# Second MLP on one core: the turn of a tile's rows moved behind the turn of the features of the tile two places ahead of it

## The chip, the cores and the metric

One core of one Trainium2 chip. The metric is the device time of one execution in microseconds (us), as the median of several runs.

## The reference

```python
def _attn_ref(r, k, v, w, u):            # (4, 8, 768, 48)
    for t in range(S):
        cur = einsum('bhd,bhe->bhde', u[None] * kt, vt)
        y[:, :, t] = einsum('bhd,bhde->bhe', rt, state + cur)
        state = wt[:, :, :, None] * state + einsum('bhd,bhe->bhde', kt, vt)

def _moe_ref(x, w_in, w_out):            # 3072 tokens, 384 -> 2048 -> 384
    h = x @ w_in
    return maximum(0.01 * h, h) @ w_out

def _moe2_ref(x, expert_emb, tau, w1, w2):   # 8 experts, 384 -> 1024 -> 384
    logits = (xn @ en.T) / tau               # xn, en: rows of unit length
    expert_idx = argmax(logits, axis=1)
    gate_w = softmax(logits)[expert_idx]
    for e in range(8):
        mask = expert_idx == e
        out[mask] = gate_w[mask, None] * (maximum(x[mask] @ w1[e], 0) @ w2[e])
```

A linear attention with decays feeds a dense MLP, and its output feeds a second MLP in which each token goes through one of eight experts. The change lies in the second MLP.

## The kernel before

Each engine has its own instruction stream, and the streams meet in semaphores. The attention and the first MLP are interleaved until about 557 us; then comes the second MLP. Its tokens are sorted by expert into tiles of 128 rows. In the profiled execution 28 tiles (0 to 27) are used. The first K1 = 5 are rows of an expert that is picked early, while the first MLP still runs. Tiles 5 to 23 stand in a loop with two tiles per turn (`tiles`, with tile 5 ahead of the loop), and tiles from NT = 24 on in nested branches (`last_tiles`), since their number depends on the data. MT = 34 is the most that there can be.

All products run as three fp32r matmuls (high x high, high x low, low x high) in place of one fp32 matmul, so every operand is split into a high and a low half: ScalarE copies the high half, VectorE subtracts it to get the low one.

One tile j goes like this:

- POOL gathers its 128 rows of 384 numbers by an indirect DMA into `xg`, which has two places (`gather`, L766, for tiles 0 to 4; `fetch`, L781, from tile 5 on). The list of rows comes into `idr` by a DMA of SP (`load_ids`, L516). A gather waits until the tile two places before has been turned (`s_xgT`).
- TensorE turns the rows with three transposes into one PSUM bank, X_BANK = 7 (`turn_g`, L1049). It waits for the gather (`s_xg`) and until the previous tile's rows have left the bank (`s_xgh`, `s_xgl`).
- ScalarE copies them to `xgh` (`x_hi2`, L1391), and VectorE makes `xgl` (`x_lo2`, L1831).
- `features(j)`: two halves of 9 matmuls of 512 columns (`feature_half`, L1067), out into the A banks. It waits for `xgh`, `xgl` and the expert's weights. ScalarE takes them out with a relu into `hs` (L1397).
- `turn_h(j)`: eight transposes (L1084) of `hs` into the H banks; ScalarE and VectorE split them into `hh` and `hl` (L1401, L1838).
- `result(j)`: 24 matmuls of 384 columns (L1103). ScalarE scales them by the gate (`scaled`, L1409) and POOL scatters them to the output (L789).

TensorE works one tile deep. Its `tile(j)` is features(j) with the turn of the rows of tile j+1 at its end, then result(j-1), then turn_h(j). ScalarE's and VectorE's `tile(j)` have x_hi2(j+1) and x_lo2(j+1) in a fixed place: behind the two relus on ScalarE, and behind the first two pieces of weights on VectorE.

Where tile j+1 has another expert than the tile two places before, SP loads its weights in four pieces into `stage` (L526), ScalarE copies the high halves (L1374) and VectorE makes the low ones (L1816): pieces 0 and 1 (for the features) at the start of tile j, pieces 2 and 3 at its end. SP loads a piece once both engines are through with the piece before it.

`start_moe` writes out tiles 0 and 1 by hand, with the last group's routing between them.

Of the kernel before, what the change touches and what calls it, by code (L numbers as in the profile page):

```python
# [23 lines left out]
def build(nc, r, k, v, w, u, w_in, w_out, emb, tau, w1, w2, out):  # L24
# [7 lines left out]
    TOK = B * S  # L32
    NT = TOK // P
    E, _, F2 = w1.shape
    FT2 = F2 // P
    GT = 3
# [4 lines left out]
    MT = K1 + (TOK - EARLY_GROUPS * GN // E + E * (P - 1)) // P  # L41
# [13 lines left out]
    with ctx:  # L55
# [299 lines left out]
        def whole(j):  # L355

            return isinstance(j, int)
# [64 lines left out]
        def routes(first, G):  # L422

            return G if first == 0 else EARLY_GROUPS - 1 + G
# [452 lines left out]
        def _(pe):  # L877
# [141 lines left out]
            def rank(r, bk, col):  # L1019

                pe.wait_ge(s_oh, r + 1)
                pe.matmul(bank[bk][:, col:col + GT * E], tri[:], r8[3][:].rearrange("p n e -> p (n e)"), start=True, stop=True)
                pe.matmul(bank[bk][:, col + GT * E:col + 2 * GT * E], ones[:], r8[3][:].rearrange("p n e -> p (n e)"),
                          start=True, stop=True).then_inc(s_rm, 1)

            def turn_x2(g, banks_):

                for i in range(GT):
                    pe.wait_ge(s_oe, GT * g + i + 1)
                    for k_ in range(KT):  # L1030
                        mm = pe.transpose(bank[banks_[i]][:, k_ * P:(k_ + 1) * P], x2s[:, i, k_ * P:(k_ + 1) * P], ident[:])
                    mm.then_inc(s_x2t, 1)

            def logit_sums(z, bk):

                pe.wait_ge(s_embt, 16 * KT)
                pe.wait_ge(s_x2e, GT * (z + 1))
                for i in range(GT):
                    for k_ in range(KT):
                        mm = pe.matmul(bank[bk][:, F_LOGIT + i * E:F_LOGIT + (i + 1) * E], x2T[:, i, k_ * P:(k_ + 1) * P],  # L1040
                                       embT[:, k_, :], start=(k_ == 0), stop=(k_ == KT - 1), skip_group_check=True)
                mm.then_inc(s_lgm, 1)

            def turn_g(j, s_, half):
                pe.wait_ge(s_xg[s_], 16 * (half + 1))
                pe.wait_ge(s_xgh, j)
                pe.wait_ge(s_xgl, j)
                for k_ in range(KT):
                    mm = pe.transpose(bank[X_BANK][:, k_ * P:(k_ + 1) * P], xg[:, s_, k_ * P:(k_ + 1) * P], ident[:])  # L1049
                mm.then_inc(s_xgT, 1)  # L1050

            def feature_half(j, s_, a):

                early_ = whole(j) and j < K1
                (w1h, w1l), _ = views(eh, el) if early_ else expert(s_)
                pe.wait_ge(s_xgh, j + 1)
                pe.wait_ge(s_xgl, j + 1)
                if early_:
                    pe.wait_ge(s_phi, a + 1)
                    pe.wait_ge(s_plo, a + 1)  # L1060
                else:
                    pe.wait_ge(s_ehi, 4 * (j - K1) + a + 1)
                    pe.wait_ge(s_elo, 4 * (j - K1) + a + 1)
                pe.wait_ge(s_hs, 2 * j)
                for k_ in range(KT):
                    for n_, (x_, w_) in enumerate(((xgh, w1h), (xgh, w1l), (xgl, w1h))):
                        mm = pe.matmul(bank[A_BANK[a]][:], x_[:, k_, :], w_[:, a, k_, :],  # L1067
                                       start=(k_ == 0 and n_ == 0), stop=(k_ == KT - 1 and n_ == 2))
                mm.then_inc(s_h2, 1)

            def features(j, s_, half):

                feature_half(j, s_, 0)
                feature_half(j, s_, 1)
                if not whole(j) or j + 1 < MT:
                    turn_g(j + 1, 1 - s_, half + s_)

            def turn_h(j):
                for a in range(2):
                    pe.wait_ge(s_hs, 2 * j + a + 1)  # L1080
                    pe.wait_ge(s_hhi, 2 * j)
                    pe.wait_ge(s_hlo, 2 * j)
                    for f in range(4):
                        mm = pe.transpose(bank[H_BANK[a]][:, f * P:(f + 1) * P], hs[:, a, f * P:(f + 1) * P], ident[:])  # L1084
                    mm.then_inc(s_hT, 1)

            def result(j, s_):
                early_ = whole(j) and j < K1
                _, (w2h, w2l) = views(eh, el) if early_ else expert(s_)
                if not whole(j) or j > 1:  # L1090
                    pe.wait_ge(s_o2e, j - 1)
                for a in range(2):
                    pe.wait_ge(s_hhi, 2 * j + a + 1)
                    pe.wait_ge(s_hlo, 2 * j + a + 1)
                    if early_:
                        pe.wait_ge(s_phi, a + 3)
                        pe.wait_ge(s_plo, a + 3)
                    else:
                        pe.wait_ge(s_ehi, 4 * (j - K1) + a + 3)
                        pe.wait_ge(s_elo, 4 * (j - K1) + a + 3)  # L1100
                    for f in range(4 * a, 4 * a + 4):
                        for n_, (h_, w_) in enumerate(((hh, w2h), (hh, w2l), (hl, w2h))):
                            mm = pe.matmul(bank[R_BANK[s_]][:, 0:DM], h_[:, f, :], w_[:, f, :],  # L1103
                                           start=(f == 0 and n_ == 0), stop=(f == FT2 - 1 and n_ == 2))
                mm.then_inc(s_o2, 1)

            def tile(j, s_, half):

                features(j, s_, half)
                result(j - 1, 1 - s_)  # L1110
                turn_h(j)

            def mlp(first, lo, hi):
                for n in range(lo, hi):
                    G, f = place(first, n)
                    if G < NG:
                        if first and f == 0:
                            turn_x(G)
                        feature(first, n)
                    if not first:  # L1120
                        for m in at(sum_at, n):
                            sums(m)
                        for m in at(turn_w_at, n):
                            turn_w(m)
                        for m in at(turn_at, n):
                            turn_rk(m)
                        for m in at(score_at, n):
                            scores(m)
                    if f == 2 and 2 <= G < NG:
                        pe.wait_ge(s_g0, n)  # L1130
                        rank(routes(first, G) - 2, *route_bank(first, G, n))
                    if G == NG - 1:
                        if f == 2:
                            turn_x2(n // FT - 1, TURN6)
                        if f == 4:
                            logit_sums(0, LOGIT6)
                        if f == 7:
                            rank(routes(first, G) - 1, *route_bank(first, G, n))
                        if f == 12:
                            turn_g(0, 0, 0)  # L1140
                    if n >= lo + LAG or (not first and n >= LAG):
                        out_part(n - LAG)
                    if not first and n == SECOND - 2:
                        pe.wait_ge(s_vs, 1)
                        pe.wait_ge(s_yhi, NC)
                        pe.wait_ge(s_ylo, NC)
                        pe.matmul(bank[STEADY[2]][:, 0:1], ones[:], violsum[:], start=True, stop=True
                                  ).then_inc(s_vt, 1)

            def start_moe(first, hi):  # L1150

                feature_half(0, 0, 0)
                turn_x2((hi - LAG) // FT - 1, TURN7)
                feature_half(0, 0, 1)
                turn_g(1, 1, 0)
                logit_sums(1, LOGIT7)
                turn_h(0)
                features(1, 1, 0)
                rank(routes(first, NG - 1), RANK7, F_LOGIT + GT * E)
                result(0, 0)  # L1160
                turn_h(1)
                for j in range(2, K1):
                    tile(j, j % 2, j // 2)

# [38 lines left out]
            def all_tiles():  # L1203

                n_used = used_tiles(pe)
                tiles(pe, tile)
                last_tiles(pe, n_used, lambda j: tile(j, j % 2, j // 2), lambda n: result(n - 1, (n - 1) % 2))
# [833 lines left out]
```

## Time and profile before

| | us |
|---|---|
| median of 3 runs | 840.05 (839.87 to 840.52) |
| the profiled execution | 839.8 |
| its span, first to last instruction | 838.0 |
| TensorE busy in the span | 820.6 |

The profiled execution's time is its span and 1.8 us around it. Times in the rows count from the start of the span. PE is TensorE's matmuls, PEld its weight loads, DVE is VectorE, ACT is ScalarE, POOL is GpSimd, SP is SyncE. Matmuls are pipelined: the time from one start to the next is what one costs, and it is less than the duration shown.

### The profile page before, as it was taken

The page shows a single profiled execution, that of the slowest core. Times are in us where ns is not written, and L with a number is a line of the kernel's source. Part 1 is how long each engine was busy: PE and PEld are TensorE (multiplying, and loading weights), DVE is VectorE, ACT ScalarE, POOL GpSimd, SP SyncE. Part 2 cuts the span into 40 slices and gives each one's busy share as a digit, 9 for nine tenths or more (in the row PEclk, how much of TensorE's full clock was granted, in tenths as well). Part 3 has the DMA queues.
Part 4 walks back from the last instruction along what each step waited for, and adds up shares of the span by engine and source line. Part 5 has one row for each costly group of instructions (what it writes and reads, how often), then busy time and mean ns, then how long its engine had stood idle before and what let it go on. Part 6 is the DMA issues. An engine that isn't in the chain of part 4 may idle for free.

```text
span 838.0 us, 17878 instructions
## 1 busy us (share of the span) xinstructions
PE 820.6 (98%) x5709; PEld 770.7 (92%) x5709; DVE 547.8 (65%) x1296; ACT 439.9 (52%) x924; POOL 203.8 (24%) x286
## 2 busy tenths in 40 slices
PE   6999999999999999999999999999999999999996
PEld 5899999999999999999999999999989998898896
DVE  6888687678789688779778755636462512545463
ACT  5675464364464475465446435554563533565573
POOL 5511111121103012112112001312363323334423
PEclk9999999999999999999999999999999999999999
DMA  9991121264231221132110001514531512475382
GB/s 206 233 240 37 39 70 35 52 101 61 54 67 39 41 70 38 39 70 51 38 25 31 1 15 31 169 38 121 181 124 38 185 47 94 138 257 202 109 295 62
DMA packets 141289, 78.52 MB, mean 94 GB/s; under 512 B 111470, under 2 KB 129237, under 8 KB 141074
## 3 DMA queue, kind: packets, MB, share of 16 engines
q1 hardware_dynamic: 132386, 64.79, 30.2%
q0 software_dynamic: 4544, 10.85, 4.0%
q10 hardware_dynamic: 4272, 1.82, 1.0%
q8 instruction: 43, 0.70, 0.4%
q14 instruction: 44, 0.36, 0.2%
HBM read 112.90 MB, written 11.63 MB: 149 GB/s over the span
## 4 chain that ended last, share of the span: by engine, by line
PE 91%; ACT 2%; issue 2%; SPq 2%; DVE 1%; DMA 1%; POOL 0%; DVEq 0%; ACTq 0%; POOLq 0%
PE bank L1015 24%; PE bank L994 23%; PE bank L1067 13%; PE bank L1103 13%; PE bank L887 3%; PE bank L920 3%; PE bank L948 3%; PE bank L1084 3%; PE bank L943 2%; PE bank L928 1%; PE bank L1049 1%; PE bank L957 1%; SPq L439 1%; DMA stage<-in_moe_w_dram 1%; DMA wraw<-in_moe_w_in_dram 1%
## 5 line engine op out<-in xcount | busy, mean ns | idle before, releaser
L994 PE MATMUL bank<-xhl,WRh 128*128 128x384 f32 x768 | 218.3, 338 | 0.2 <-issue 0.2
L1360 ACT COPY gw<-bank 128x384 f32<-128x384 f32 x128 | 61.6, 481 | 158.7 <-PE bank L994 158.4
L994 PEld LDWEIGHTS bank<-xhl,WRh 128*128 128x128 f32 x768 | 141.2, 188 | 0.4 <-issue 0.4
L1015 PE MATMUL bank<-WRh,gh 128*128 128x384 f32 x384 | 136.4, 355 | 0.0
L994 PE MATMUL bank<-xhl,WRl 128*128 128x384 f32 x384 | 130.1, 339 | 0.0
L1015 PE MATMUL bank<-WRh,gl 128*128 128x384 f32 x384 | 129.7, 338 | 0.0
L1015 PE MATMUL bank<-WRl,gh 128*128 128x384 f32 x384 | 129.6, 337 | 0.0
L1663 DVE SCALAR_TENSOR_TENSOR gw<-gw 128x384 f32<-128x384 f32 x128 | 72.9, 570 | 62.1 <-ACT gw L1360 62.1
L1670 DVE TENSOR_TENSOR gl<-gw,gh 128x384 fp32r<-128x384 f32 x128 | 78.9, 616 | 47.2 <-ACT gh L1366 44.9
L1366 ACT CAST gh<-gw 128x384 fp32r<-128x384 f32 x128 | 65.4, 511 | 70.5 <-DVE gw L1663 58.2
L1838 DVE TENSOR_TENSOR hl<-bank,hh 128x512 fp32r<-128x512 f32 x56 | 36.1, 686 | 84.8 <-ACT hh L1401 84.5
L714 POOL TENSOR_TENSOR St<-Sx,FL 128x256 f32<-128x256 f32 x20 | 12.3, 614 | 292.4 <-DVE Sx L1644 229.7
L1683 DVE CUSTOM_DVE_ANT_0 junk<-x2s,embb 128x384 bf16<-128x384 f32 x144 | 76.5, 574 | 0.0
L1015 PEld LDWEIGHTS bank<-WRh,gh 128*128 128x128 f32 x384 | 72.3, 188 | 1.4 <-issue 0.7
L1015 PEld LDWEIGHTS bank<-WRl,gh 128*128 128x128 f32 x384 | 72.4, 189 | 0.0
L1816 DVE TENSOR_TENSOR WRl<-stage,WRh 128x1536 fp32r<-128x1536 f32 x36 | 61.8, 1756 | 15.9 <-ACT WRh L1374 15.9
L994 PEld LDWEIGHTS bank<-xhl,WRl 128*128 128x128 f32 x384 | 72.2, 188 | 0.0
L1015 PEld LDWEIGHTS bank<-WRh,gl 128*128 128x128 f32 x384 | 72.1, 188 | 0.0
L1103 PE MATMUL bank<-WRh,hh 128*128 128x384 f32 x184 | 63.9, 347 | 1.1 <-DVEq L1827 1.1
L1409 ACT ACTIVATE os<-bank,gcol 128x384 f32<-128x384 f32 x28 | 16.3, 583 | 88.1 <-PE bank L1103 88.1
L1103 PE MATMUL bank<-WRl,hh 128*128 128x384 f32 x184 | 62.0, 337 | 0.0
L1103 PE MATMUL bank<-WRh,hl 128*128 128x384 f32 x184 | 61.9, 336 | 0.0
(196 smaller groups left out, 1635.5 us busy)
## 6 DMA issues: line engine op xcount, KB each, us to landing
stage<-in_moe_w_dram SPq DMA_DIRECT2D x96, 768.0 KB
Wn<-in_w_dram SPq DMA_DIRECT2D x24, 192.0 KB, 2.7
Kn<-in_k_dram SPq DMA_DIRECT2D x24, 192.0 KB, 3.5
Vn<-in_v_dram SPq DMA_DIRECT2D x24, 192.0 KB, 3.1
x_moe<-x2s SPq DMA_DIRECT2D x24, 192.0 KB, 2.7
Rn<-in_r_dram SPq DMA_DIRECT2D x21, 192.0 KB, 3.4
wraw<-in_moe_w_out_dram SPq DMA_DIRECT2D x4, 768.0 KB, 7.3
eraw<-in_moe_w_dram SPq DMA_DIRECT2D x4, 768.0 KB, 8.8
```

Source lines behind the costliest of these rows:

```text
L887: mm = pe.transpose(bank[bk][:, h * P:(h + 1) * P], src[:, m % NSLOT, 2 * h:2 * h + 2, :].rearrange("p h d -> p (h d)"), ident[:])
L994: mm = pe.matmul(bank[F_BANK[n % 2]][:, 0:GN], win(t_)[:, f // 4, k_, cols], xhl[G % 2][:, a, k_, :], start=(k_ == 0 and n_ == 0), stop=(k ...
L1015: mm = pe.matmul(bank[O_BANK[i]][:, 0:DM], a[:, z, cols], wout(t_)[:, f, :], start=(f == 0 and n_ == 0), stop=(f == FT - 1 and n_ == 2))
L1067: mm = pe.matmul(bank[A_BANK[a]][:], x_[:, k_, :], w_[:, a, k_, :], start=(k_ == 0 and n_ == 0), stop=(k_ == KT - 1 and n_ == 2))
L1103: mm = pe.matmul(bank[R_BANK[s_]][:, 0:DM], h_[:, f, :], w_[:, f, :], start=(f == 0 and n_ == 0), stop=(f == FT2 - 1 and n_ == 2))
L1360: act.copy(gw[:, n % 2, :], bank[F_BANK[n % 2]][:, 0:GN]).then_inc(s_g0, 1)
L1366: act.copy(gh[:, n % GS, :], gw[:, n % 2, :]).then_inc(s_ghi, 1)
L1663: dve.scalar_tensor_tensor(gw[:, z, :], gw[:, z, :], 0.01, gw[:, z, :], ALU.mult, ALU.max).then_inc(s_g1, 1)
L1670: dve.tensor_tensor(gl[:, n % GS, :], gw[:, n % 2, :], gh[:, n % GS, :].bitcast(F32), ALU.subtract).then_inc(s_glo, 1)
L1683: dve.tensor_tensor_reduce(junk[:, m % 2, :], x2s[:, i, :], embb[:, e, :], 1.0, 0.0, ALU.mult, ALU.add, logits[:, GT * G + i, e:e + 1]).th ...
L1816: dve.tensor_tensor(sel(w1l, w2l), src, sel(w1h, w2h).bitcast(F32), ALU.subtract).then_inc(s_elo, 1)
L1838: dve.tensor_tensor(lo, bank[H_BANK[a]][:], hi.bitcast(F32), ALU.subtract).then_inc(s_hlo, 1)
```

## The change

In TensorE's stream alone, the turn of rows leaves its place between `features` and `result`. It now stands behind `turn_h(j)` and turns the rows of tile j+2. For tiles from NT on, where it is not known whether there is a next tile, it stands in front of the features and turns tile j+1, which is the same place in the sequence. In `start_moe` the turn of rows 2 stays where it was, and that of rows 3 moves up behind turn_h(1).

```diff
@@ features @@
                 feature_half(j, s_, 0)
                 feature_half(j, s_, 1)
-                if not whole(j) or j + 1 < MT:
-                    turn_g(j + 1, 1 - s_, half + s_)
@@ tile @@
+                maybe_last = whole(j) and j >= NT
+                if maybe_last and NT < j < MT - 1:
+                    turn_g(j + 1, 1 - s_, half + s_)
                 features(j, s_, half)
                 result(j - 1, 1 - s_)
                 turn_h(j)
+                if not maybe_last:
+                    turn_g(j + 2, s_, half + 1)
@@ start_moe @@
                 features(1, 1, 0)
+                turn_g(2, 0, 1)
                 rank(routes(first, NG - 1), RANK7, F_LOGIT + GT * E)
                 result(0, 0)
                 turn_h(1)
+                turn_g(3, 1, 1)
```

## Rows read from the trace of the kernel before

**Rows 1.** The page: busy time of an engine, and TensorE's granted clock in 40 slices.
```profile
PE 820.6 (98%) x5709; PEld 770.7 (92%) x5709; DVE 547.8 (65%) x1296; ACT 439.9 (52%) x924; POOL 203.8 (24%) x286
...
PEclk9999999999999999999999999999999999999999
```
**Rows 2.** Busy us (and instructions) of each engine by stretch, granted clock, DMA share, GB/s.
```profile
594.59:604.09 9.50, 9.50 (x57) 8.67 (x55) 5.18 (x5) 5.86 (x9) 3.41 (x6) 1.00 0.45 146
...
748.35:758.53 10.18, 9.84 (x56) 8.70 (x55) 8.52 (x7) 8.99 (x13) 5.73 (x5) 1.00 0.79 268
...
562.50:565.60 3.10, 3.10 (x30) 3.06 (x29) 0.77 (x3) 2.60 (x5) 1.05 (x1) 1.00 0.00 0
```
**Rows 3.** Waits from 590 us on: waiter, releaser, us in total, times, longest.
```profile
PEld bank L1067 <- issue: 2.5, 4, 0.9
...
PEld bank L1103 <- issue: 1.4, 1, 1.4
```
**Rows 4.** Timeline of a steady tile on TensorE: start, us, line, operation, count.
```profile
704.47 0.40 PE L1067 MATMUL bank<-WRh,xgl 128*128 128x512 f32 x1
704.71 0.49 PE L1049 MATMUL bank<-ident,xg 128*128 128x128 f32 x3
704.95 0.42 PE L1103 MATMUL bank<-WRh,hh 128*128 128x384 f32 x1
705.21 0.34 PE L1103 MATMUL bank<-WRl,hh 128*128 128x384 f32 x1
...
709.22 1.03 PE L1084 MATMUL bank<-ident,hs 128*128 128x128 f32 x8
710.01 0.48 PE L1067 MATMUL bank<-WRh,xgh 128*128 128x512 f32 x1
710.33 0.40 PE L1067 MATMUL bank<-WRl,xgh 128*128 128x512 f32 x1
```
**Rows 5.** Timeline of POOL: the gathers of tiles 4, 5, 6 and 18.
```profile
578.48 1.20 POOL L766 DMA_INDIRECT xg<-x_moe,idall  x1 [0.16 <-issue]
...
592.24 1.07 POOL L781 DMA_INDIRECT xg<-x_moe,gi  x1 [0.92 <-POOL gi L777]
...
597.93 1.85 POOL L781 DMA_INDIRECT xg<-x_moe,gi  x1 [0.92 <-POOL gi L777]
...
706.07 1.06 POOL L781 DMA_INDIRECT xg<-x_moe,gi  x1 [0.91 <-PE bank L1049]
```
**Rows 6.** Gathers, issue to landing: tile 4's, 5's, 6's, and all 26 of L781.
```profile
DMA to landing us min/median/max: 7.8/7.8/7.8
...
DMA to landing us min/median/max: 3.2/3.2/3.2
...
DMA to landing us min/median/max: 6.2/6.2/6.2
...
DMA to landing us min/median/max: 3.0/3.2/8.1
```
**Rows 7.** Timeline of SP's queue: the first four pieces of expert weights.
```profile
578.04 3.28 SPq L526 DMA_DIRECT2D stage<-in_moe_w_dram  x4
```
**Rows 8.** Timeline of TensorE: the ends of tiles 2, 3 and 4.
```profile
584.30 1.03 PE L1084 MATMUL bank<-ident,hs 128*128 128x128 f32 x8
...
593.80 1.03 PE L1084 MATMUL bank<-ident,hs 128*128 128x128 f32 x8
...
603.30 1.03 PE L1084 MATMUL bank<-ident,hs 128*128 128x128 f32 x8
```
**Rows 9.** Timeline around the wait in front of tile 21's features.
```profile
754.19 3.42 DVE L1816 TENSOR_TENSOR WRl<-stage,WRh 128x1536 fp32r<-128x1536 f32 x2
...
757.15 1.03 PE L1084 MATMUL bank<-ident,hs 128*128 128x128 f32 x8
...
757.53 0.55 DVE L1831 TENSOR_TENSOR xgl<-bank,xgh 128x384 fp32r<-128x384 f32 x1
...
758.53 0.49 PE L1067 MATMUL bank<-WRh,xgh 128*128 128x512 f32 x1 [0.35 <-issue]
```

## The prediction

> **What bounds the kernel now.** I read the page first: TensorE is busy for 98% of the span at the full granted clock [rows 1]. Then the busy time by stretch of the second MLP: an ordinary tile lasts 9.50 us and TensorE is busy in all of it, a tile with late expert weights lasts 10.18 us with 9.84 us busy [rows 2]. Then the list of waits from 590 us to the end: TensorE's weight loads stand still in front of the features (L1067) 4 times, 2.5 us together, and once more, 1.4 us, in front of the last result [rows 3]. So TensorE's own instructions set the end. Whatever the change gives or takes on them counts in full, and a new wait on TensorE counts in full too, unless a later one of those five takes it back.
>
> **What the change moves.** No instruction is added or removed: tiles 0 to 28 have their rows turned before and after, three transposes each. Before, tile j runs features(j), turn of rows j+1, result(j-1), turn_h(j). After, it runs features(j), result(j-1), turn_h(j), turn of rows j+2. So eleven transposes stand together, and each turn of rows comes earlier by one result and one turn_h. Two things follow. What a block of transposes costs beyond its transposes is paid once a tile instead of twice. And the gathered rows must have landed 5.1 us earlier than now: a result (24 x 0.174 = 4.2) and a turn_h (0.9), both from [rows 4].
>
> **The saving per tile.** The steady tile [rows 4] shows starts. The block of three begins at 704.71, the result at 704.95; the first result matmul takes 0.26 us to the second, where the other 23 take (709.22 - 705.21) / 23 = 0.174. Cost of the block: 0.24 + 0.26 - 0.17 = 0.33 us, 0.11 per transpose. The block of eight: 709.22 to 710.01 is 0.79, the first feature matmul takes 0.32 instead of about 0.235, together 0.875 us, 0.109 per transpose. The longer first matmul behind a block (0.09) is thus paid for by the last transpose, which takes only some 0.03 to the next start (0.79 - 7 x 0.109): a switch costs next to nothing. Eleven transposes cost 11 x 0.109 = 1.20 against 0.33 + 0.875 = 1.21 us. I take 0.01 us a tile; about 20 of the tiles lie where it isn't swallowed by a wait: **-0.2 us**. The bounds are 0 and, if each block of three really cost its 0.09, 26 x 0.09 = 2.3 us.
>
> The block of eleven lasts 1.2 us. A stretch of 3.1 us that was nothing but transposes and 8-column matmuls ran at clock 1.00, the upper of the two levels, and so did the tiles around it [rows 2], so I take nothing for the clock. The Trainium skill (TensorE: Matmul & The Clock Gate, Part 4: PE-mode transpose) says that transposes do not count as busy for the clock. If eleven in a row dropped it to 1.2 GHz and cost only their own doubling, that would be 26 x 1.2 = 31 us; the trace speaks against it, and it is a rival below.
>
> **Are the rows there in time?** In the steady part, yes: the gather issued at 706.07 is tile 18's [rows 5], and its new turn comes behind turn_h(16), one tile of 9.6 us after turn_h(15) at 709.22 [rows 4], so at 719.7. Gathers land 3.2 us after issue in the median and 8.1 at most [rows 6], so by 714.2. At the start it is tighter, since the first gathers stand behind the routing. Tile 4's gather is issued at 578.48 [rows 5] and lands 7.8 us later [rows 6], at 586.28. It stands beside the first four pieces of expert weights, 768 KB each, which SP issues from 578.04 on [rows 7]; later gathers land in 3.2. Before, its turn came behind features(3), 18 x 0.235 = 4.2 us into tile 3. After, it comes right behind turn_h(2), which starts at 584.30 and is over at 584.30 + 0.875 = 585.17 [rows 8]. TensorE waits 586.28 - 585.17 = 1.1 us, and some 0.1 until the first transpose goes. Behind that wait in TensorE's queue stand the five waits of features(3), which no longer run ahead; the three transposes (0.33 us) cover most of them, I take 0.1. **+1.3 us.** Its bounds: 0 if the gather came in 3.2 us, and 2.2 if it came 0.5 us later and nothing of the waits were covered (0.4).
>
> By the Trainium skill (DMA: Bandwidth & Descriptors, Queues, rings and completion order) each DMA engine takes turns between its queues, packet by packet, so a gather on POOL's queue should not stand behind SP's weights. By this rule it would land in about 3 us; the 7.8 us of [rows 6] go against it. This is a rival too.
>
> Tile 5's gather is issued at 592.24 and lands 3.2 us later, at 595.44 [rows 5, 6]. It waits for its row list, not for TensorE, so it does not move. Its turn is wanted behind turn_h(3): 593.80 + 0.88 = 594.67 [rows 8], plus the delay of 1.3, 595.97. No further wait, but without the first it would cost 0.8. Tile 6's gather follows result(2), so it moves with TensorE: 597.93 + 6.2 = 604.13 against turn_h(4)'s end at 603.30 + 0.88 = 604.18, both plus 1.3. That is even to 0.05 us; a little of it would be taken back by the wait in front of features(6). Later ones have room.
>
> **The four waits in front of the features.** They are in front of tiles 6, 21, 23 and 27 by the timeline. In the one at 758.5, tile 21's [rows 9], VectorE works through its splits of expert weights and only then makes xgl (757.53 + 0.55 = 758.08); the features start 0.45 us later, which is TensorE's sequencer with the waits that stood behind. That chain starts from turn_h two tiles before. Since the rows' turn in the middle of the tile is gone, turn_h comes 0.33 us earlier relative to the features, so the chain ends 0.33 us earlier. But the turn of rows j+2 waits for the same xgl (one bank, X_BANK) and now stands between it and the features: +0.33 if nothing overlaps, +0.2 if its transposes run under the 0.45 us of sequencer time, +0.5 where the loop's entry comes in between too (tile 6). Three of the four chains are independent (tiles 6, 21, 27; tile 23's starts from the same turn_h as tile 21's ends). I take +0.2, -0.1 and +0.1: **+0.15 us** in all, bounds -1.0 and +0.6. The wait in front of the last result is untouched: turn_h(27), ScalarE's copy, VectorE's subtraction follow each other as before.
>
> **Bookkeeping of the moved turn.** Features(2) starts 0.33 us late, as rows 3 are turned ahead of it, and the last tile gives that back, since no turn stands behind features(27). Nothing in all. ScalarE's copy of the rows (x_hi2) stands behind both relus as before and finds its input ready. POOL's gather waits for the turn two tiles before; it can only start earlier.
>
> **Sum.** -0.2 + 1.3 + 0.15 = +1.25 us on the profiled execution's 839.8, 841.05. The median of the runs is 0.25 above that execution, so 841.3.
>
> **The rivals.**
> 1. *Forecast*: one new wait of about 1.2 us ahead of features(3), the rest even. 841.3, own range 840.6 to 842.0. Chance 0.60.
> 2. *The chains' 0.33 us stay saved*: the transposes hide under the sequencer's 0.45 us. 840.05 + 1.3 - 0.2 - 1.0 = 840.15. For it: the 0.45 us is there in three of the waits. Against: the features' own waits are still behind the transposes in the queue. 0.13.
> 3. *Tile 4's gather is early, tile 5's waits instead*: 0.8 + 0.15 - 0.2, 840.8. 0.07.
> 4. *More gathers late*: tile 6's lands 7.8 us after issue like tile 4's, 1.6 us later than now; 1.5 wait, 0.5 taken back in front of features(6): 842.3. It decides from any landing above 6.3 us. 0.13.
> 5. *Other side, faster*: a switch costs TensorE its 0.09 us on the way in and on the way out, 26 x 0.18 = 4.7 us saved, less 1.45: 836.8. It gets under 838.4 from 0.12 us a tile on. Against: blocks of three and of eight cost the same per transpose. 0.06.
> 6. *The clock falls in the block of eleven*: +31 us, 871. 0.01.
>
> **Numbers.** A measurement of this kernel can tell about 0.2%, 1.7 us, from no change: 838.4 to 841.7. Faster: rival 5, 0.06. Slower: rivals 4 and 6 and about a fifth of the first, 0.27. Within: 0.67. Range 839.4 to 842.7: it takes in cases 1 to 4 with their bounds and leaves out 5, 6 and the far ends.
>
> **What would show it.** In the new profile TensorE stands still some 1.2 us ahead of its transposes L1049 near 585.2, where it now has none; the transposes stand as 8 + 3, with one longer matmul behind them; a steady tile is 0.01 us shorter; the waits in front of tiles 6, 21, 23 and 27 end with xgl, then three transposes, then the features. The forecast is wrong if tile 4's rows land before 585.2, if a steady tile changes by over 0.05 us (26 times 0.05 is 1.3), or if waits appear ahead of L1049 in the steady part, which would mean that the gathers have less room than I worked out.

## The result

The changed kernel takes 841.82 us (median of 12 runs, 840.89 to 843.75) against 840.29 us of the kernel before, run beside it; the ratio is 1.002, with a 95% interval of 1.0012 to 1.0027. That is 1.5 us slower by the medians (1.0 to 2.3 by the interval), at the edge of what can be told from no change. The forecast was 841.3, 1.25 us over its base. A second measurement (e10 below) gave 1.0017 (1.0008 to 1.0026).

In the profile after, the page's chain that ended last has one entry that the kernel before does not have, the gather that fetches rows by `idall`:

```profile
PE bank L1015 24%; PE bank L994 22%; PE bank L1067 13%; PE bank L1101 13%; PE bank L887 3%; PE bank L920 3%; PE bank L948 3%; PE bank L1082 2%; PE bank L943 2%; PE bank L928 1%; PE bank L1049 1%; PE bank L957 1%; DMA xg<-x_moe,idall 1%; SPq L439 1%; DMA wraw<-in_moe_w_in_dram 1%
```

(turn_h is now L1082 and the result L1101.) TensorE's timeline at the end of tile 2, to hold against [rows 8]: the eight transposes start at 584.66, the rows' three only at 586.98, with the gather named as what was waited for.

```profile
584.66 1.03 PE L1082 MATMUL bank<-ident,hs 128*128 128x128 f32 x8
586.98 0.55 PE L1049 MATMUL bank<-ident,xg 128*128 128x128 f32 x3 [1.29 <-DMA xg<-x_moe,idall]
587.28 0.47 PE L1067 MATMUL bank<-eh,xgh 128*128 128x512 f32 x1
```

Without a wait L1049 would have started 0.87 us behind 584.66, at 585.53: the wait is 1.45 us. POOL issued that gather at 578.83, and it landed 8.1 us later (7.8 in [rows 6]); SP's weights had started 0.46 us ahead of it:

```profile
578.83 1.19 POOL L766 DMA_INDIRECT xg<-x_moe,idall  x1 [0.16 <-issue]
```
```profile
DMA to landing us min/median/max: 8.1/8.1/8.1
```
```profile
578.37 1.60 SPq L526 DMA_DIRECT2D stage<-in_moe_w_dram  x3
```

At the end of tile 4 there is a small wait for tile 6's rows (0.2 us) and a larger one behind it, which the forecast does not have: three transposes at 606.26, the features only at 607.14, 0.88 us later where 0.25 is usual.

```profile
605.20 1.03 PE L1082 MATMUL bank<-ident,hs 128*128 128x128 f32 x8
606.26 0.55 PE L1049 MATMUL bank<-ident,xg 128*128 128x128 f32 x3
607.14 0.48 PE L1067 MATMUL bank<-WRh,xgh 128*128 128x512 f32 x1 [0.33 <-issue]
```

The view of line 368 shows why. TensorE's sequencer (PEldq) reads the number of used tiles there once, between tiles 4 and 5. In the kernel after it does so at 606.3, when the turn in front has just been released; in the kernel before at 601.6, under the result's matmuls. The first two rows are of after, the last one of before.

```profile
L368 PEldq TENSOR_LOAD <-used x1: 310/310/310, 606.3 to 606.3; - x1
...
L368 PEldq FUSED_REGOPS  x1: 156/156/156, 606.6 to 606.6; - x1
```
```profile
L368 PEldq TENSOR_LOAD <-used x1: 314/314/314, 601.6 to 601.6; - x1
```

A steady tile, to hold against [rows 4]. The result now starts without a longer first matmul (0.17 to the second), and the block is 8 + 3 transposes with one longer matmul behind it (712.46 to 712.78):

```profile
707.18 0.34 PE L1101 MATMUL bank<-WRh,hh 128*128 128x384 f32 x1
707.35 0.34 PE L1101 MATMUL bank<-WRl,hh 128*128 128x384 f32 x1
...
711.34 1.04 PE L1082 MATMUL bank<-ident,hs 128*128 128x128 f32 x8
712.22 0.49 PE L1049 MATMUL bank<-ident,xg 128*128 128x128 f32 x3
712.46 0.48 PE L1067 MATMUL bank<-WRh,xgh 128*128 128x512 f32 x1
712.78 0.40 PE L1067 MATMUL bank<-WRl,xgh 128*128 128x512 f32 x1
```

The wait in front of tile 21, to hold against [rows 9]: xgl ends at 759.63 + 0.55 = 760.18, then the three transposes, then the features 0.57 us behind xgl, where it was 0.45.

```profile
759.23 1.03 PE L1082 MATMUL bank<-ident,hs 128*128 128x128 f32 x8
...
759.63 0.55 DVE L1836 TENSOR_TENSOR xgl<-bank,xgh 128x384 fp32r<-128x384 f32 x1
...
760.32 0.52 PE L1049 MATMUL bank<-ident,xg 128*128 128x128 f32 x3
...
760.75 0.50 PE L1067 MATMUL bank<-WRh,xgh 128*128 128x512 f32 x1
```

The following table comes from the timelines. It counts each tile's first feature matmul from that of tile 0 (557.41 in before, 557.75 in after) and subtracts the same count in the first profile of the kernel before. Columns t3 to t27 are those tiles, "result" is the first matmul of the last result, and the last column is the mean length of tiles 8 to 19 in us. Rows e1 to e12 are the experiments below.

```
us later than before   t3     t4     t5     t6     t20    t21    t27   result  steady tile
after                 +1.86  +1.87  +2.71  +2.21  +2.07  +1.88  +1.41  +1.20   9.577
before (absolute)     27.68  37.18  46.68  56.74 190.95 201.12 260.16 271.11   9.587
e1  late start         0.00   0.00   0.00  +0.49  +0.36  +0.18  -0.28  -0.58   9.577
e2  only start        +1.50  +1.71  +2.10  +1.39  +1.38  +2.02  +1.48  +1.48   9.587
e3  gather 4 early    +0.35  +1.48  +1.46  +1.46  +1.34  +1.14  +0.78  +0.47   9.577
e4  lists first       +0.35  +0.37  +1.21  +0.70  +0.54  +0.35  -0.18  -0.51   9.577
e5  three blocks      +0.04  +0.09  +0.12  +0.12  -0.14  -0.13  -0.50  -0.51   9.567
e6  used early        +1.41  +1.77  +1.76  +1.76  +1.63  +1.44  +1.43  +1.13   9.577
e7  lists + used      +0.35  +1.59  +1.59  +1.63  +1.50  +1.30  +0.89  +0.59   9.577
e8  before again       0.00   0.00   0.00   0.00   0.00  +0.01  -0.43  -0.41   9.587
e9  four blocks       +0.10  +0.13  +0.21  +0.20  +0.13  +0.13  -0.12  -0.11   9.580
e10 after again       +0.35  +1.23  +1.24  +1.40  +1.27  +1.08  +0.93  +0.63   9.577
e11 lists, before      0.00   0.00   0.00   0.00  -0.01   0.00  -0.20  -0.19   9.587
e12 four again        +0.10  +0.13  +0.50  +0.49  +0.41  +0.42  +1.15  +1.18   9.580
```

The profile after is 2.0 us longer than that of before. Of this 0.34 lies ahead of tile 0, where the kernels are the same, 1.20 between tile 0 and the last result, and 0.45 behind the last result's start (9.97 against 9.52 us). The kernel before, profiled again (e8), takes 10.05 us there. So only the middle one belongs to the change, and single profiles stray by some tenths at each of the other places. The middle one strays too: the first profile of before had a wait in front of tile 27 that its second one (e8) has not. Against e8 the profile after is 1.61 us longer between tile 0 and the last result, and the second profile of the changed kernel (e10) 1.04.

### The profile page after: what moved, and what is told of

It reads as the page before. It is cut to its first block, busy times and chain, and to the rows that moved or that the text cites. A ratio compares the mean times of both kernels' runs of the same rounds, so it can differ in the third digit from the quotient of the medians.

```text
span 840.0 us, 17878 instructions
## 1 busy us (share of the span) xinstructions
PE 821.4 (98%) x5709; PEld 772.1 (92%) x5709; DVE 547.8 (65%) x1296; ACT 440.4 (52%) x924; POOL 203.0 (24%) x286
## 4 chain that ended last, share of the span: by engine, by line
PE 90%; DMA 2%; ACT 2%; issue 2%; SPq 1%; DVE 1%; POOL 0%; DVEq 0%; ACTq 0%; POOLq 0%
PE bank L1015 24%; PE bank L994 22%; PE bank L1067 13%; PE bank L1101 13%; PE bank L887 3%; PE bank L920 3%; PE bank L948 3%; PE bank L1082 2%; PE bank L943 2%; PE bank L928 1%; PE bank L1049 1%; PE bank L957 1%; DMA xg<-x_moe,idall 1%; SPq L439 1%; DMA wraw<-in_moe_w_in_dram 1%
## 5 line engine op out<-in xcount | busy, mean ns | idle before, releaser
L1101 PE MATMUL bank<-WRh,hh 128*128 128x384 f32 x184 | 62.0, 337 | 1.3 <-DVEq L1832 1.3
L1101 PE MATMUL bank<-WRh,hl 128*128 128x384 f32 x184 | 61.9, 336 | 0.0
L1101 PE MATMUL bank<-WRl,hh 128*128 128x384 f32 x184 | 61.9, 336 | 0.0
```

## The experiments

All ratios are to the kernel before, run beside the experiment on the same chip.

**e1: the old place at the start, the new one from tile 5 on.**

```diff
@@ start_moe @@
                 turn_h(1)
-                turn_g(3, 1, 1)
@@ tile @@
                 features(j, s_, half)
+                if whole(j) and j <= K1:
+                    turn_g(j + 1, 1 - s_, half + s_)
                 result(j - 1, 1 - s_)
                 turn_h(j)
-                if not maybe_last:
+                if not maybe_last and not (whole(j) and j < K1):
                     turn_g(j + 2, s_, half + 1)
```

> The changed kernel with the old place of the turn (between features and result) for tiles 2 to 5 and the new place from tile 5 on. Theory, the cost is made at the start: the wait for tile 4's rows (1.5 us in the changed kernel) and the 0.6 us in front of features(5) are gone, the wait in front of features(6) is back (0.5 us or a little more), steady tiles stay at 9.577 us. Time within 0.3 us of the kernel before, ratio 1.000. Rival, the cost is spread over the steady tiles or lies in the chains of late weights: still about 1.5 us over the kernel before, ratio 1.002.

Measured: 839.79 us, ratio 0.9996 (0.9987 to 1.0005), as the first theory has it. Tiles 3 to 5 start as in the kernel before. In front of tile 6 stand 1.0 us where there were 0.5: the one turn that is paid here anyway, and TensorE's entry into its loop behind the wait for xgl.

**e2: the new place for rows 3 to 6 alone, on the kernel before.**

```diff
@@ features @@
-                if not whole(j) or j + 1 < MT:
+                if (not whole(j) or j + 1 < MT) and not (whole(j) and j <= K1):
                     turn_g(j + 1, 1 - s_, half + s_)
@@ tile @@
                 turn_h(j)
+                if whole(j) and j < K1:
+                    turn_g(j + 2, s_, half + 1)
```

(and turn_g(2), turn_g(3) in `start_moe` as in the change.)

> The kernel before with the new place for the turns of rows 3 to 6 alone (none in tile 5, the old place from tile 6 on). Theory, the cost is made at the start: the same 1.5 us wait for tile 4's rows and 0.6 us in front of features(5), 0.5 us taken back in front of features(6), steady tiles at 9.587 us as before, so nothing saved later: 1.6 to 2.0 us over the kernel before, ratio 1.002. Rival: within 0.4 us of the kernel before.

Measured: 842.07 us, ratio 1.002 (1.001 to 1.003). The loss is there with the start alone, and steady tiles keep their 9.587 us. TensorE's waits name the gather of tile 4:

```profile
PE bank L1049 <- DMA xg<-x_moe,idall: 0.9, 1, 0.9
```

Features(3) start 1.50 us late; without the 0.33 of the turn that moved ahead this is a wait of 1.2 us where 1.5 were expected. In front of features(5) stand 0.4 us where 0.6 were expected, and tile 5's rows, too, were a little late (0.15 us). The wait ahead of tile 21 was 1.2 us here, 0.6 in the kernel before, with the same code there: a piece of weights landed later.

**e3: tile 4's gather issued behind tile 3's.**

```diff
                 tile(0, 0, 0)
+                gather(4)
                 scatter(first, NG - 1, routes(first, NG - 1))
```

(and not in tile 1.)

> The changed kernel with POOL's gather of tile 4 issued right behind that of tile 3, some 8 us earlier and ahead of the expert weights. Theory: it lands in about 3 us, TensorE's wait in front of tile 3 goes; tile 5's rows, which land at the same time as now, are then 0.8 us late with some 0.1 for the sequencer, and tile 6's are as late as now: 0.5 to 0.7 us under the changed kernel, 0.8 to 1.0 over the kernel before, ratio 1.001. Rival, the wait only hides another one of the same length: as slow as the changed kernel.

Measured: 841.04 us, ratio 1.0013 (1.0004 to 1.0022). The wait in front of tile 3 is gone and the one for tile 5's rows has come, by the waits 0.9 us on TensorE's matmuls and 1.05 by the starts (0.8 + 0.1 were expected):

```profile
PEld bank L1051 <- DMA xg<-x_moe,gi: 1.1, 1, 1.1
...
PE bank L1051 <- DMA xg<-x_moe,gi: 0.9, 1, 0.9
```

The time is 1.0 us under e2's 842.07, measured on the same chip. Against the changed kernel's ratios of 1.0020 and 1.0017 its 1.0013 lies within the intervals. So the trace shows that the wait moved; that this gains time is only suggested.

**e4: SP's first two row lists ahead of the weights.**

```diff
-                weights(K1)
                 sp.wait_ge(s_rows, 1)
                 sp.wait_ge(s_tab, 16 * GT * (routes(first, NG - 1) + 1))
                 load_ids(K1, 1)
                 load_ids(K1 + 1, 0)
+                weights(K1)
                 load_ids(K1 + 2, 1)
```

> The changed kernel with SP's first two row lists ahead of the first expert weights, which start some 4 us later. Theory, the weights are what the gathers of tiles 4 and 5 stand behind: tile 4's gather lands in 3 to 4 us and tile 5's some 5 us earlier than now, both waits go, the weights are still there in time. What stays is the 0.6 us in front of features(5) and the wait for tile 6's rows: 0 to 0.4 us over the kernel before, ratio 1.000. Rival, the gather is slow for itself (its issue 0.3 us behind the copies, 8 us to landing whatever runs beside it): the wait in front of tile 3 stays at 1.5 us.

Measured: 840.63 us, ratio 1.0007 (0.9998 to 1.0016). The weights start at 584.58, tile 4's gather at 579.17 as before. Neither tile 3 nor tile 4 waits. So tile 4's gather is slow because of the weights, not for itself. (The trace of e4 has no landing for it; that of e7, with the same order of transfers, has one, 3.8 us after issue.) What stays is the 0.8 us ahead of features(5).

```profile
581.68 1.45 SPq L516 DMA_DIRECT2D idr<-token_lists  x2
584.58 2.42 SPq L526 DMA_DIRECT2D stage<-in_moe_w_dram  x4
```

**e5: the turn of rows cut in two blocks, on the kernel before.** The calls, in `features`; `turn_g` takes the transposes that it is to set, waits ahead of the first of the three and signals behind the last.

```diff
                 feature_half(j, s_, 0)
+                if not whole(j) or j + 1 < MT:
+                    turn_g(j + 1, 1 - s_, half + s_, range(0, 1))
                 feature_half(j, s_, 1)
                 if not whole(j) or j + 1 < MT:
-                    turn_g(j + 1, 1 - s_, half + s_)
+                    turn_g(j + 1, 1 - s_, half + s_, range(1, KT))
```

> The kernel before with its turn of rows cut in two: one transpose between the two halves of the features, two behind them. The same transposes, three blocks a tile instead of two. Theory, a switch between matmuls and transposes costs next to nothing: a steady tile gets 0.00 to 0.02 us longer, the time stays within 0.6 us of the kernel before, ratio 1.000 to 1.001. Rival, each block costs its longer first matmul, 0.09 us on one side or 0.18 us on both: 2.4 or 4.7 us slower, ratio 1.003 or 1.006.

Measured: 839.80 us, ratio 0.9992 (0.9983 to 1.0000); a steady tile takes 9.567 us, 0.02 less than with two blocks. The rival is refuted, and the theory's sign was off too. The single transpose's timeline:

```profile
664.58 0.39 PE L1069 MATMUL bank<-WRh,xgl 128*128 128x512 f32 x1
664.81 0.27 PE L1050 MATMUL bank<-ident,xg 128*128 128x128 f32 x1
664.84 0.47 PE L1069 MATMUL bank<-WRh,xgh 128*128 128x512 f32 x1
665.15 0.39 PE L1069 MATMUL bank<-WRl,xgh 128*128 128x512 f32 x1
```

The next matmul starts 0.03 us behind it and is 0.08 us longer: 0.11 us, as in any block.

**e6: TensorE's read of the number of used tiles ahead of tile 4.** The part in `start_moe`; behind it the number is handed on to the later tiles instead of being read there.

```diff
@@ start_moe @@
-                for j in range(2, K1):
+                for j in range(2, K1 - 1):
                     tile(j, j % 2, j // 2)
+                n_used = used_tiles(pe)
+                tile(K1 - 1, (K1 - 1) % 2, (K1 - 1) // 2)
+                return n_used
```

> The changed kernel with TensorE's read of the number of used tiles one tile earlier, ahead of tile 4 instead of behind it. Theory, the 0.6 us ahead of features(5) is that read, its branch checks and the waits behind it, which stand behind the wait for tile 6's rows in TensorE's queue: it shrinks to under 0.2 us, and part comes back in front of features(6), so 0.2 to 0.6 us under the changed kernel. Rival, it is the expert weights of tile 5 that are late: the 0.6 us stays.

Measured: 841.81 us, ratio 1.0011 (1.0003 to 1.0020), against the changed kernel's 1.0020 and 1.0017; the intervals overlap. In the trace the 0.6 us ahead of features(5) is gone, so it was the read and what stands behind it. But 0.34 us of it now stands ahead of features(4), since there, too, the sequencer had no lead (L1049 at 596.97, features at 597.56), and the wait in front of tile 6 is back with 0.5. At tile 6 nothing is left of the gain: from the start of features(3) to that of features(6) both kernels take 29.41 us.

```profile
596.97 0.49 PE L1049 MATMUL bank<-ident,xg 128*128 128x128 f32 x3
597.56 0.47 PE L1067 MATMUL bank<-eh,xgh 128*128 128x512 f32 x1
```

**e7: e4 and e6 together.**

> The changed kernel with both edits: SP's first two row lists ahead of the expert weights, and TensorE's read of the number of used tiles one tile earlier. Theory: no wait in front of tiles 3 and 4, at most 0.3 us in front of tile 5, about 0.5 us in front of tile 6; from there the saving of 0.01 us a tile: within 0.4 us of the kernel before, ratio 0.999 to 1.0005. Rival, the start alone does not account for the loss: over 1 us slower than the kernel before.

Measured: 840.92 us, ratio 1.0004 (0.9996 to 1.0013). The ratio is within what was expected (the medians are 0.44 us apart, and 0.4 was the limit), the trace isn't. In front of tile 4, 1.2 us are lost: tile 5's gather now met the later weights and took 6.7 us, and the read stands behind it.

```profile
589.57 1.07 POOL L781 DMA_INDIRECT xg<-x_moe,gi  x1 [0.92 <-POOL gi L777]
```
```profile
DMA to landing us min/median/max: 6.7/6.7/6.7
```

**e8: the kernel before, profiled once more.** No edit.

> The kernel before once more, for one profile. Theory, the waits in front of tiles 21, 23 and 27 depend on when pieces of weights land and differ from one execution to the next by some tenths of a microsecond with the same code: at least one of them differs from the first profile by 0.2 us or more. Rival, they are the same to 0.05 us, and then the 0.5 us that the changed kernel has less in front of tile 27 comes from the new order.

Measured: 840.11 us in its one run. Tiles 1 to 21 start within 0.02 us of the first profile. The wait in front of tile 27 (0.59 us) is gone: there the copies of four pieces of weights follow each other without a gap, while in the first profile the last of them waited 1.3 us for its landing. TensorE's waits in front of features are three instead of the four of [rows 3]:

```profile
PEld bank L1067 <- issue: 2.0, 3, 0.9
```

So the 0.5 us that the changed kernel had less in front of tile 27 is an accident of the first profile of before.

**e9: the three transposes of rows one by one, four blocks a tile.** On the kernel before: one behind each half of the features, one in the middle of the result. The calls of `turn_g`, without the conditions around them and without the new argument of `result`:

```diff
@@ features @@
                 feature_half(j, s_, 0)
+                    turn_g(j + 1, 1 - s_, half + s_, range(0, 1))
                 feature_half(j, s_, 1)
-                    turn_g(j + 1, 1 - s_, half + s_)
+                    turn_g(j + 1, 1 - s_, half + s_, range(1, 2))
@@ result @@
+                    if a == 0 and rows is not None:
+                        turn_g(*rows, range(2, 3))
```

> The kernel before with its three transposes of rows set one by one: behind the first half of the features, behind the second half, and in the middle of the result. Four blocks a tile instead of two. Theory, a single transpose between matmuls costs less than one in a block (0.105 against 0.109 us): a steady tile under 9.57 us, against 9.587 before and 9.567 with three blocks, and 0.3 to 1.0 us under the kernel before in all, ratio 0.999. Rival, three blocks were an accident of where the matmuls start: a steady tile back at 9.58 us or over.

Measured: 841.42 us, ratio 1.0016 (1.0007 to 1.0025), with a steady tile of 9.580 us. The rival has it: more blocks save nothing, and three blocks' 9.567 does not carry on. The profile did not show where the 1.6 us (841.42 against 839.85 of the kernel before) went: its second MLP was as long as before, but its first 25 us were 1.25 us longer, in code that is the same.

**e10: the changed kernel once more.** No edit.

> The changed kernel once more, on the same chip as the four-block kernel. Theory: 1.2 to 1.7 us over the kernel before; in the profile the wait for tile 4's rows is 1.0 to 1.6 us and 0.6 us stand in front of features(5); from tile 6 on every steady tile takes 9.577 us; the waits in front of tiles 21, 23 and 27 differ from the first profile by up to 0.5 us, as the landings of weights do. Rival: the wait for tile 4's rows was an accident of one execution and is under 0.5 us.

Measured: 841.52 us, ratio 1.0017 (1.0008 to 1.0026). The time repeats, the place does not: what was written down as the run's rival, tile 4's rows waiting less than 0.5 us, is what happened. Tile 4's rows are there in time; tile 5's are late instead, 0.8 us by the starts, as in e3:

```profile
584.47 1.03 PE L1082 MATMUL bank<-ident,hs 128*128 128x128 f32 x8
585.34 0.49 PE L1049 MATMUL bank<-ident,xg 128*128 128x128 f32 x3
```
```profile
593.99 1.03 PE L1082 MATMUL bank<-ident,hs 128*128 128x128 f32 x8
595.66 0.55 PE L1049 MATMUL bank<-ident,xg 128*128 128x128 f32 x3 [0.64 <-DMA xg<-x_moe,gi]
```

Here SP's weights start at 579.00, 0.37 us behind POOL's gather at 578.63; in the profile above they start 0.46 us ahead of theirs. This is what rival 3 of the forecast describes. And the 0.6 us ahead of features(5) is missing, since tile 6's rows now came without a wait and the read stayed under the result.

```profile
579.00 0.02 SPq L526 DMA_DIRECT2D stage<-in_moe_w_dram  x1
```

The order at the issue does not settle which rows are late. In e2 the weights started 0.41 us behind the gather of tile 4, as here, and its rows were 1.2 us late all the same:

```profile
579.33 1.20 POOL L766 DMA_INDIRECT xg<-x_moe,idall  x1 [0.15 <-issue]
...
579.74 2.70 SPq L526 DMA_DIRECT2D stage<-in_moe_w_dram  x4
```

**e11: e4's edit on the kernel before.**

> The kernel before with SP's first two row lists ahead of the expert weights. Theory, the order of these transfers matters only where rows are turned early: within 0.4 us of the kernel before, ratio 1.000, no wait in front of tiles 3 to 5. Rival, the later weights themselves cost or save something: a change of over 0.8 us either way.

Measured: 840.34 us, ratio 1.0005 (0.9996 to 1.0014), no wait in front of tiles 3 to 5. The order of the transfers matters only where rows are turned early.

**e12: the four-block kernel once more.**

> The four-block kernel once more. Its profile had the second MLP as long as the kernel before (0.1 us less from the first feature to the last result) but the first 25 us of the program 1.25 us longer, where the two kernels are the same. Theory, that start is an accident of single executions: the ratio falls back to 0.999 to 1.001, and the first 200 matmuls are less than 0.6 us behind. Rival, it belongs to this kernel: ratio 1.0015 again, and the first 25 us longer by over 1 us again.

Measured: 841.92 us, ratio 1.0023 (1.0013 to 1.0032). The slow first 25 us did not come back (0.14 us), so they were an accident; the loss did, and its cause stays open. In this profile it lies at tile 22, 1.2 us longer than in the kernel before, and 0.4 us at tile 4. In both profiles POOL's gathers wait for the transpose that moved into the result, which the kernel before shows only 3 times, 2.7 us:

```profile
POOL xg L781 <- PE bank L1050: 39.1, 18, 3.9
```

Later gathers share the DMA engines with the weights at other times. That they delay the piece of tile 23 was not tested by itself. This profile shows one thing more: SP's weights started at 579.56 here, 1.05 us behind the gather of tile 4 at 578.51, and that gather landed after 4.0 us:

```profile
DMA to landing us min/median/max: 4.0/4.0/4.0
```

## Why the forecast held, point by point

- **The new wait.** Forecast: 1.2 us for tile 4's rows, +1.3 with what stands behind it. In the first profile after it was 1.45 us, with 0.06 for the first transpose and next to nothing for the features' waits. Features(3) start 1.86 us late, 0.33 of which is the turn that moved ahead: 1.53. e2 makes the loss with the start alone and e1 takes it away, which shows the place. e4 shows the cause, the weights: with them 5.4 us behind the gather the wait is gone.
- **It is not always that wait.** The forecast put rival 3 (tile 5's rows late instead, 840.8) at 0.07. e10 is that case: features(6) start 1.40 late instead of 2.21. By the forecast's own sign (tile 4's rows there before 585.2) its mechanism does not hold in e10's profile, though the time repeats. The kernels that turn rows 4 early and issue gather and weights as before had tile 4's rows late by 1.45 us (after), 1.2 (e2), 1.1 (e6) and 0 (e10), and tile 5's by 0, 0.15, 0 and 0.8. The weights started 0.46 us ahead of the gather in after and 0.44 in e6, and 0.37 and 0.41 us behind it in e10 and e2. So a lead of 0.4 us for the gather is not enough by itself; what decides there, and how often each case comes, stays open.
- **Tile 6's gather**, forecast as even to 0.05 us: it landed 6.4 us after issue instead of 6.2, so the rows were 0.2 us late in the first profile, and that was taken back in front of features(6), as forecast. What the forecast missed is the read of the number of used tiles that stands behind that wait in TensorE's queue: 0.6 us. I had listed the waits behind the gather and not looked for what else the sequencer does between tiles 4 and 5. Of the 0.85 us the wait in front of tile 6 took back 0.5, so 0.35 stays; e6 removed it and gained nothing by tile 6, since the chain of weights then ends last. In place of the 0.15 us that the four chains were to cost, tiles 4 to 6 cost 0.35 by themselves here, 0.17 in e10.
- **The chains of late weights.** turn_h comes 0.33 us earlier relative to the features, and the turn stands between xgl and the features. At tile 21 the chain's copies start 0.32 us earlier in after (0.64 instead of 0.96 us behind features(20)) and 0.12 is given back: -0.2, forecast -0.1, the same in e1, e3, e4, e6, e7 and e10. At tile 6 e1 measured +0.49 with the 0.33 of the turn in it, so +0.16; forecast +0.17. At tile 27 the profile after shows -0.48, and the forecast was +0.1. By e8 that is the landing of one piece in the first profile of before: against e8, tile 26 is 9.69 instead of 9.70 us, even to 0.01. Single profiles are no measure for these waits.
- **The saving per tile** was forecast at 0.01 us and measured at 0.010 (9.577 against 9.587), in every kernel with the new order. Rival 5, that a switch costs 0.09 or 0.18, is refuted by e5 and e9: with one, two, three and four blocks a tile takes 9.577, 9.587, 9.567 and 9.580 us. The times do not rise with the number of blocks; what makes their 0.02 us was not found.
- **The clock** stayed at 1.00 in the block of eleven, so rival 6 is out. The Trainium skill (TensorE: Matmul & The Clock Gate, Part 4: PE-mode transpose) says that transposes do not count as busy in the same way; no run here shows an effect of that on the clock. These are the changed kernel's stretches of tile 4 and of tile 8: busy us of each engine, then clock.

```profile
596.79:607.14 10.35, 9.99 (x56) 8.77 (x55) 5.84 (x7) 6.69 (x11) 3.70 (x7) 1.00 0.53 182
635.85:645.43 9.58, 9.58 (x57) 8.72 (x55) 1.85 (x3) 3.12 (x7) 2.72 (x6) 1.00 0.14 41
```

- **Queues that take turns.** By the Trainium skill (DMA: Bandwidth & Descriptors, Queues, rings and completion order) each DMA engine takes turns between its queues, packet by packet; the forecast drew from it that the gather should not stand behind the weights. It lands 7.8 to 8.1 us after issue beside them in before and after, and 3.8 us in e7, with the weights 5.4 us behind it. The measurement decides: the weights cost this gather 4.0 to 4.3 us, and tile 5's gather in e7, which met the later weights, 3.5 (6.7 against 3.2).
- **The sum** of +1.25 us came out as +1.5 and +1.7 by the medians, with a better hit than its terms, and that is luck in part: the wait with what stands behind it was 0.2 us larger than forecast in one profile and 0.4 smaller in the other, the read was missing, and the chains were taken too high at tile 21. Two sums of the forecast are loose as well. Its three terms for the chains, +0.2, -0.1 and +0.1, give +0.2 and not +0.15, unless one takes them unrounded (+0.17, -0.13, +0.1). And the upper bound of the new wait is 1.1 + 0.5 + 0.1 + 0.4 = 2.1 us, not 2.2. Neither moves the forecast by more than 0.1 us.

e1 and e5 are the fastest kernels of the study, at 0.9996 and 0.9992. Neither is beyond 0.2%, so no version was found that clearly beats the kernel before.

## What to carry to other kernels

Asking for data one stage earlier costs nothing in the steady part, where buffers give slack, and can cost a microsecond or more at the start of a stage, where the first transfers run beside others: look up the landing of each of the first few transfers against its new due time. When an engine gets a new wait, list all that stands behind it in its queue, reads of values and branches included. Here they added 0.6 us in one place. A saving that is read from a longer first matmul behind a block must be set against the last one of the block, which is shorter by as much.

## What the runs showed of the hardware

- A gather on POOL beside four loads of 768 KB on SP, issue to landing: 7.7 to 8.1 us when the loads started 0.44 to 0.46 us first (before, after, e5, e6, e8), 4.0 us when they started 1.05 us behind it (e12), 3.8 us at 5.4 us behind (e7). With the loads 0.4 us behind it came in time in e10 (under 6.7 us) and 1.2 us late in e2, so there something else decides.
- A block of n fp32 transposes between fp32r matmuls cost n x 0.11 us from start to start, for n of 1, 2, 3, 8 and 11, at a granted clock of 1.00, the upper level.
- A sequencer's read of one value (0.31 us, and 0.3 of register work and waits behind it) cost TensorE nothing while it ran ahead, and 0.6 us once it had caught up (after, tile 4; 0.34 us in e6).
